# Sixteen drains on GpSimd's queue taken out of a fused attention and mixture-of-experts kernel

## The chip, the cores and the metric

The kernel runs on one core of a Trainium2 chip. Its time is device microseconds of one execution; a measurement is the median of several. A core has four computing engines, each with its own queue of instructions: TensorE (PE, matmul), VectorE (DVE), ScalarE (ACT) and GpSimd (POOL); SyncE (SP) issues transfers. The engines wait for one another by semaphores, and the program sets each of these waits by hand.

## The reference

```
scores = z @ z^T / S                       # per batch, B = 8, S = 3072, 64 features
attn   = max(scores, 0) ** 2
x      = u * (attn @ v)                    # (B*S, 256)
# mixture of experts, E = 8, capacity = 768, F = 1024
expert = argmax(x @ w_gate);  gate = softmax probability of that expert
# the first 768 tokens of an expert, in order, get a place; the others give zero rows
h = max(disp[e] @ w1[e], 0);  y = h @ w2[e]
out[token] = gate * y[its place]
```

## The kernel before

The work has two stages.

The first stage goes over groups of 384 tokens (three tiles of 128). For each group TensorE makes scores and the weighted sums of v, ScalarE and VectorE turn scores into squared weights in two half-precision parts, and the group is routed: VectorE works out each token's place in the buffer `disp`, and GpSimd writes the three tiles of rows there with three indirect DMAs (scatters, line 358). The stage stops early, by a flag that every engine reads, as soon as all experts are full; in these runs that is after 18 groups, so after 54 scatters. In each turn GpSimd waits for the group's places, issues the three scatters, reads the flag, waits until the scatters have landed (`scattered`, line 375) and goes on.

The second stage is a loop of four turns over pairs of experts; each turn has four blocks k = 0 to 3, a block being 384 rows of `disp`. SP loads a block's rows by a transposing DMA and its tail (gate factor and token number) by a plain one (lines 321 and 323), four blocks ahead at first and then each as soon as the scatters of the block that used the buffer have landed (`y_scattered`, line 336). TensorE multiplies by w1 and w2. ScalarE evacuates a block's three result tiles (line 536) and counts `y_ready`; GpSimd waits for each and scatters the tile to `out` (line 393), three scatters for a block and 48 in all. In blocks k = 1 and 3 of the first three turns GpSimd also does an all-reduce over partitions ahead of the scatters (line 388).

Of the kernel before, what the change touches and what calls it, by code (L numbers as in the profile page):

```python
# [40 lines left out]
def relu2_attention_moe(nc, u, v, z, w_gate, w1, w2, out, disp, capacity):  # L41
    B, S, D = u.shape
    DQK = z.shape[2]
    E, _, F = w1.shape
    NG = B * GPB
    DC = D // P
# [10 lines left out]
    with ExitStack() as ctx:  # L57
# [139 lines left out]
        def wait_apart(eng, semaphore, value):  # L197

            eng.wait_ge(semaphore, value)
            if not isinstance(value, int):  # L200
                eng.sem_inc(s["passed"], 1)

        def only_if(eng, cond, step):
            if isinstance(cond, bool):
                if cond:
                    step()
            else:
                with eng.If(cond):
                    step()

        def attention_loop(eng, body):

            end = eng.alloc_register(f"end_{eng.engine.name}")
            eng.reg_mov(end, NG + 1)
            body(0, end)
            with eng.Fori(1, end) as n:
                body(nc.s_assert_within(n, 1, NG), end)

        def load_end(eng, n, end):  # L220

            if isinstance(n, int):
                return
            wait_apart(eng, s["flag_ready"], n)
            eng.reg_load(end, ends[0:1, bass.ds((n - 1) & (NG - 1), 1)])
# [114 lines left out]
        @block.gpsimd  # L340
        def _(pool):
            pool.wait_ge(s["nrm0"], 1)
            pool.partition_all_reduce(amx[:, 0:1], mx[:, 0:1], P, RMAX).then_inc(s["amx0"], 1)
            pool.wait_ge(s["vsum0"], 1)
            pool.partition_all_reduce(amx[:, 1:2], mx[:, 1:2], P, RMAX).then_inc(s["amx0"], 1)
            pool.wait_ge(s["gmx_ready"], 1)
            pool.partition_all_reduce(gamx[:, :], gmx[:, :], P, RMAX).then_inc(s["gamx_ready"], 1)

            def body(n, end):
                g = n & 7  # L350
                if isinstance(n, int):

                    pool.wait_ge(s["disp_filled"], 16 * 8)
                    pool.sem_inc(s["row_free"], 1)
                    return
                wait_apart(pool, s["slot_ready"], n * 2)
                for t in range(TILES):
                    pool.indirect_dma_start(  # L358
                        out=disp[:, :], out_offset=bass.IndirectOffsetOnAxis(ap=slot[:, t:t + 1], axis=0),
                        in_=xrow[:, t, :], in_offset=None, bounds_check=E * capacity - 1, oob_is_err=False,  # L360
                    ).then_inc(s["scattered"], 16)

                def reduce_maxes():
                    wait_apart(pool, s["maxes_ready"], (n & 120) + 8)
                    pool.partition_all_reduce(amx[:, :], mx[:, :], P, RMAX).then_inc(s["allmax_ready"], 8)
                load_end(pool, n, end)
                def all_w(e):
                    pool.wait_ge(s["wmax_ready"], e + 1)
                    pool.partition_all_reduce(wamx[:, :], wmx[:, :], P, RMAX).then_inc(s["wallmax_ready"], 1)

                def rest():
                    only_if(pool, g == 3, reduce_maxes)
                    only_if(pool, n == 8, lambda: all_w(0))
                    only_if(pool, n == 9, lambda: all_w(1))
                wait_apart(pool, s["scattered"], n * 48)
                pool.sem_inc(s["row_free"], 1)
                only_if(pool, pool.snap(end) > 0, rest)
            attention_loop(pool, body)
            pool.drain()
            pool.wait_ge(s["out_zeroed"], 16 * 8)  # L380

            with pool.Fori(0, E // 2) as i:
                for k in range(4):
                    j = i * 4 + k
                    if k % 2:
                        def all_w():
                            wait_apart(pool, s["wmax_ready"], i * 2 + k // 2 + 3)
                            pool.partition_all_reduce(wamx[:, :], wmx[:, :], P, RMAX).then_inc(s["wallmax_ready"], 1)
                        only_if(pool, i < E // 2 - 1, all_w)
                    for at, t in enumerate(BANK_ORDER):  # L390

                        wait_apart(pool, s["y_ready"], j * TILES + TILES + at + 1)
                        pool.indirect_dma_start(  # L393
                            out=out, out_offset=bass.IndirectOffsetOnAxis(
                                ap=tail[:, k, t, 1:2].bitcast(U32), axis=0),
                            in_=ybuf[:, k % 2, t, :], in_offset=None, bounds_check=B * S - 1, oob_is_err=False,
                        ).then_inc(s[f"y_scattered{k}"], 16)
                    only_if(pool, True if k < 3 else i < E // 2 - 1, lambda: pool.drain())
            for k in range(4):
                pool.wait_ge(s[f"y_scattered{k}"], 16 * TILES * E * HALVES // 4)  # L400

# [891 lines left out]
```

## Time and profile before

| | us |
|---|---|
| median of 3 runs | 894.89 |
| lowest and highest | 893.61 and 895.44 |
| the profiled execution | 893.61 |
| its span, first to last instruction | 891.8 |

| engine | busy us | share of the span |
|---|---|---|
| TensorE, matmul | 871.2 | 98% |
| VectorE | 644.3 | 72% |
| ScalarE | 567.0 | 64% |
| GpSimd | 121.5 | 14% |

### The profile page before, as it was taken

Reading aid. Unit: us, or ns where it says so; the run is one execution under the profiler, and the core shown is the slowest. Engines: PE = TensorE matmul, PEld = TensorE weight load, DVE = VectorE, ACT = ScalarE, POOL = GpSimd, SP = SyncE. Lnnn points to the kernel's source line nnn. Section 1 sums busy time; section 2 is a strip of 40 time slices with the busy share of each in tenths; the row PEclk is TensorE's granted clock in tenths of the full one; section 3 lists DMA queues with packets and bytes.
Section 4 is the critical chain, followed back from the end, with each engine's and each line's share of the span. In section 5 each row is a group of like instructions: output and inputs, shape, how many; then the busy total and the mean of one; then the engine's idle time right before and its main releaser. Section 6 shows DMA issues by size and latency. Waiting matters only on the chain.

```text
span 891.8 us, 23154 instructions
## 1 busy us (share of the span) xinstructions
PE 871.2 (98%) x7573; PEld 701.0 (79%) x7574; DVE 644.3 (72%) x1393; ACT 567.0 (64%) x869; POOL 121.5 (14%) x120
## 2 busy tenths in 40 slices
PE   5999999999999999999999999999899999999997
PEld 4787888888888888888888888888677777777775
DVE  7976877988988988889888797677255565655531
ACT  6868786767777679886776777677144344434422
POOL 0001102101101110110110110110112112121212
PEclk9999999999999999999999999999999999999999
DMA  9973528623632740010111112400715245325101
GB/s 269 209 232 129 177 70 295 194 93 101 194 127 67 238 147 7 34 35 18 35 40 31 35 51 61 143 24 18 167 40 149 54 129 165 98 79 152 51 19 36
DMA packets 123207, 93.93 MB, mean 105 GB/s; under 512 B 59453, under 2 KB 118026, under 8 KB 123184
## 3 DMA queue, kind: packets, MB, share of 16 engines
q1 hardware_dynamic: 118288, 80.99, 32.7%
q0 software_dynamic: 4896, 12.64, 4.0%
q8 instruction: 14, 0.23, 0.1%
q14 instruction: 9, 0.07, 0.0%
HBM read 40.03 MB, written 44.93 MB: 95 GB/s over the span
## 4 chain that ended last, share of the span: by engine, by line
PE 95%; DMA 1%; DVE 1%; issue 1%; ACT 0%; POOL 0%; POOLq 0%; SPq 0%; DVEq 0%
PE O L621 16%; PE O L625 16%; PE O L623 16%; PE Sc L740 14%; PE Sc L589 8%; PE Sc L590 8%; PE O L761 5%; PE O L763 5%; PE O L765 5%; PE M L662 1%; DMA vS<-disp 1%; PE M L670 1%; DMA rawz<-in_z 1%; DVE zsq L863 0%; DVE zsq L868 0%
## 5 line engine op out<-in xcount | busy, mean ns | idle before, releaser
L623 PE MATMUL O<-vS,attn_hi 128*128 128x256 f16 x1326 | 361.8, 273 | 0.0
L621 PE MATMUL O<-vS,attn_hi 128*128 128x256 f16 x1326 | 361.7, 273 | 0.0
L625 PE MATMUL O<-vS,attn_lo 128*128 128x256 f16 x1326 | 361.7, 273 | 0.0
L431 ACT ACTIVATE Sc<-Sc 128x768 f32<-128x768 f32 x223 | 177.3, 795 | 78.6 <-PE Sc L590 65.1
L902 DVE TENSOR_TENSOR attn_lo<-attn,attn_hi 128x768 f16<-128x768 f32 x223 | 213.8, 959 | 7.7
L435 ACT ACTIVATE attn<-Sc 128x768 f32<-128x768 f32 x223 | 180.9, 811 | 7.1
L621 PEld LDWEIGHTS O<-vS,attn_hi 128*128 128x128 f16 x1326 | 129.8, 98 | 26.7 <-issue 0.2
L623 PEld LDWEIGHTS O<-vS,attn_hi 128*128 128x128 f16 x1326 | 129.8, 98 | 26.6 <-issue 0.2
L589 PE MATMUL Sc<-zPQ 128*128 (+1 forms) x448 | 146.9, 328 | 3.6 <-ACT attn L435 2.7
L590 PE MATMUL Sc<-zPQ 128*128 (+1 forms) x448 | 147.0, 329 | 0.0
L896 DVE CAST attn_hi<-attn 128x768 f16<-128x768 f32 x223 | 124.4, 558 | 28.0 <-ACT attn L435 22.8
L1206 DVE SCALAR_TENSOR_TENSOR rawv<-Sc,rawv 128x768 f16<-128x768 f32 x64 | 61.2, 956 | 114.3 <-ACT rawv L524 96.6
L625 PEld LDWEIGHTS O<-vS,attn_lo 128*128 128x128 f16 x1326 | 129.8, 98 | 15.3
L358 POOL DMA_INDIRECT disp<-xrow,slot x54 | 69.1, 1280 | 481.2 <-DVE slot L1076 448.0
L524 ACT ACTIVATE rawv<-Sc 128x768 f16<-128x768 f32 x64 | 51.9, 811 | 109.5 <-PE Sc L740 106.2
L740 PE MATMUL Sc<-vS,w1h 128*128 128x384 f16 x512 | 104.1, 326 | 2.2 <-DMA vS<-disp 2.1
L761 PE MATMUL O<-w2s,rawv 128*128 128x256 f16 x384 | 104.7, 273 | 0.0
L763 PE MATMUL O<-w2s,rawv 128*128 128x256 f16 x384 | 104.7, 273 | 0.0
L765 PE MATMUL O<-w2s,rawv 128*128 128x256 f16 x384 | 104.7, 273 | 0.0
L740 PEld LDWEIGHTS Sc<-vS,w1h 128*128 128x128 f16 x512 | 49.9, 98 | 30.7 <-DMA vS<-disp 2.3
L393 POOL DMA_INDIRECT out<-attn,vS x48 | 47.0, 979 | 130.9 <-ACT attn L536 120.2
L589 PEld LDWEIGHTS Sc<-zPQ 128*128 128x128 f16 (+1 forms) x448 | 44.0, 98 | 22.5 <-issue 4.7
(136 smaller groups left out, 823.3 us busy)
## 6 DMA issues: line engine op xcount, KB each, us to landing
out<-empty SPq DMA_DIRECT2D x8, 3072.0 KB
wraw<-in_moe_w SPq DMA_DIRECT2D x16, 1024.0 KB
rawv<-in_v SPq DMA_DIRECT2D x16, 768.0 KB, 8.3
ubuf<-in_u SPq DMA_DIRECT2D x19, 384.0 KB, 3.2
disp<-empty SPq DMA_DIRECT2D x8, 774.0 KB, 17.0
rawz<-in_z SPq DMA_DIRECT2D x3, 768.0 KB
disp<-xrow,slot POOLq DMA_INDIRECT x54
rawz<-in_z SPq DMA_DIRECT2D x2, 384.0 KB, 4.3
```

The lines of the kernel that those rows point to most:

```text
L431: act.activation(pair, pair, ACT.Relu).then_inc(s["relu_done"], 1)
L435: act.activation(attn[:, c % BUFS, :, :], Sp[:, 2 * (c % 2):2 * (c % 2) + 2, 0:GROUP], ACT.Square, scale=ROOT_C).then_inc(s["square_done"], 1)
L589: nc.tensor.matmul(to, keys, zall[:, bass.ds(qb, GROUP)], start=True, stop=False)
L590: ins = nc.tensor.matmul(to, keys, zall[:, bass.ds(qb + SLICE * P, GROUP)], start=False, stop=True)
L621: nc.tensor.matmul(o_part(t), hi, v[:, 0:D], start=c == 0 and j == 0 and t % 2 == 0, stop=False, skip_group_check=True)
L623: nc.tensor.matmul(o_part(t), hi, v[:, D:2 * D], start=False, stop=False, skip_group_check=True)
L625: ins = nc.tensor.matmul(o_part(t), lo, v[:, 0:D], start=False, stop=c == PAIRS - 1 and j == 1, skip_group_check=True)
L740: ins = nc.tensor.matmul(Sp[:, 2 * (p % 2) + fi, 0:GROUP], w[par][:, m, f * P:(f + 1) * P], xt[:, k, x + m, :], start=(at == 0), stop=(at ...
L761: nc.tensor.matmul(o_part(t), hi, w2s[:, par, f, 0:D], start=f == 0 and t % 2 == 0, stop=False, skip_group_check=True)
L763: nc.tensor.matmul(o_part(t), hi, w2s[:, par, f, D:2 * D], start=False, stop=False, skip_group_check=True)
L765: ins = nc.tensor.matmul(o_part(t), lo, w2s[:, par, f, 0:D], start=False, stop=f == FC - 1, skip_group_check=True)
L902: dve.tensor_tensor(attn_lo[:, b, :, :], attn[:, b, :, :], attn_hi[:, b, :, :], ALU.subtract).then_inc(s["lo_done"], 1)
```

## The change

Both drains in the program's text go: the one between the stages, and the one behind each block's scatters together with its condition. All waits on semaphores stay.

```diff
--- before.py
+++ after.py
@@ -376,7 +376,6 @@
                 pool.sem_inc(s["row_free"], 1)
                 only_if(pool, pool.snap(end) > 0, rest)
             attention_loop(pool, body)
-            pool.drain()
             pool.wait_ge(s["out_zeroed"], 16 * 8)
 
             with pool.Fori(0, E // 2) as i:
@@ -395,7 +394,6 @@
                                 ap=tail[:, k, t, 1:2].bitcast(U32), axis=0),
                             in_=ybuf[:, k % 2, t, :], in_offset=None, bounds_check=B * S - 1, oob_is_err=False,
                         ).then_inc(s[f"y_scattered{k}"], 16)
-                    only_if(pool, True if k < 3 else i < E // 2 - 1, lambda: pool.drain())
             for k in range(4):
                 pool.wait_ge(s[f"y_scattered{k}"], 16 * TILES * E * HALVES // 4)
```

## Rows read from the trace of the kernel before

**Rows 1.** The page: TensorE's busy time, and the chain by engine

```profile
PE 871.2 (98%) x7573; PEld 701.0 (79%) x7574; DVE 644.3 (72%) x1393; ACT 567.0 (64%) x869; POOL 121.5 (14%) x120
...
PE 95%; DMA 1%; DVE 1%; issue 1%; ACT 0%; POOL 0%; POOLq 0%; SPq 0%; DVEq 0%
```

**Rows 2.** Stretches: from:to, length, busy by engine, clock, DMA share, GB/s

```profile
0.00:627.00 627.00, 615.27 (x5572) 508.79 (x5574) 515.03 (x1220) 465.06 (x729) 71.68 (x66) 0.99 0.37 109
...
636.00:886.00 250.00, 249.81 (x1914) 186.85 (x1912) 129.02 (x172) 101.17 (x139) 47.19 (x52) 1.00 0.35 96
886.00:891.80 5.80, 0.00 (x0) 0.00 (x0) 0.00 (x0) 0.81 (x2) 1.95 (x2) 0.75 0.19 68
```

**Rows 3.** The chain in order of time, its end: start us, us, what

```profile
885.82 0.12 PE O L765
...
887.33 0.52 POOL out L393
...
888.60 0.98 POOL out L393
```

**Rows 4.** By line, GpSimd's last waits and drains: count, ns min/median/max, first/last start

```profile
L400 POOLq EVENT_SEMAPHORE  x1: 43/43/43, 891.0 to 891.0; - x1
...
L57 POOLq DRAIN  x1: 293/293/293, 891.3 to 891.3; - x1
...
L1279 POOLq DRAIN  x1: 174/174/174, 0.3 to 0.3; - x1
```

**Rows 5.** GpSimd between the stages (timeline, then by line), and all L398 drains

```profile
626.66 0.97 POOL L358 DMA_INDIRECT disp<-xrow,slot  x1 [0.30 <-issue]
...
L201 POOLq EVENT_SEMAPHORE  x1: 17/17/17, 628.8 to 628.8; - x1
...
L379 POOLq DRAIN  x1: 4476/4476/4476, 629.4 to 629.4; - x1
...
L398 POOLq DRAIN  x15: 3368/3392/4001, 656.7 to 875.9; - x15
```

**Rows 6.** By line: three single L398 drains, and SP's waits for scatters' landing

```profile
L398 POOLq DRAIN  x1: 3377/3377/3377, 656.7 to 656.7; - x1
L201 SPq EVENT_SEMAPHORE  x1: 17/17/17, 659.9 to 659.9; - x1
...
L398 POOLq DRAIN  x1: 4001/4001/4001, 674.7 to 674.7; - x1
...
L398 POOLq DRAIN  x1: 3617/3617/3617, 688.0 to 688.0; - x1
L201 SPq EVENT_SEMAPHORE  x1: 17/17/17, 691.5 to 691.5; - x1
```

**Rows 7.** Timeline of GpSimd, second stage: start, us, what [idle before <-releaser]; one wait

```profile
653.96 0.97 POOL L393 DMA_INDIRECT out<-attn,vS  x1 [26.33 <-ACT attn L536]
...
672.15 0.36 POOL L388 PARTITION_ALL_REDUCE wamx<-wmx  x1 [13.66 <-DVE wmx L1168]
...
685.27 0.97 POOL L393 DMA_INDIRECT out<-attn,vS  x1 [8.22 <-ACT attn L536]
...
L201 POOLq EVENT_SEMAPHORE  x1: 17/17/17, 883.9 to 883.9; - x1
...
884.79 0.97 POOL L393 DMA_INDIRECT out<-attn,vS  x1 [7.06 <-ACT attn L536]
```

**Rows 8.** By line, GpSimd's scatters of either stage, ns min/median/max

```profile
L358 POOL DMA_INDIRECT disp<-xrow,slot x54: 974/1182/1528, 69.6 to 626.7; - x54
...
L393 POOL DMA_INDIRECT out<-attn,vS x48: 967/972/1027, 654.0 to 888.6; - x48
```

**Rows 9.** Seam: TensorE's wait (by waits), landing of loads issued at 629.3 and 660.1

```profile
PE Sc L740 <- DMA vS<-disp: 2.1, 1, 2.1
...
DMA to landing us min/median/max: 5.4/5.4/5.4
...
DMA to landing us min/median/max: 3.6/3.6/3.6
```

## The prediction

> **What bounds the kernel now.** I read the shares of the engines and of the chain first [rows 1]: TensorE is busy 98% of the span and 95% of the chain is TensorE, so the body of the kernel goes at the pace of the matmuls. GpSimd is busy 14%, and the edit touches GpSimd alone. The table of stretches [rows 2] says the same by stage: from 636 to 886 us TensorE is busy 249.8 of 250 us; the 5.8 us after 886 have no matmul in them. So I read two places instruction by instruction: this end, and the seam between the two stages, where TensorE waits 2.1 us once [rows 9].
>
> The end [rows 3]: the last matmul stands there until 885.94, ScalarE evacuates, GpSimd issues its second scatter at 887.33 and its third at 888.60, which ends at 889.58. The chain stops there, 2.2 us ahead of the span's end. That is the row on which this forecast hangs.
>
> **The change, part by part.** It removes L379 (one drain, 4.476 us) and L398 (15 drains, 3.37 to 4.00 us each) [rows 5], with the condition around the one in k = 3, and adds nothing.
>
> *What the drains cost where they stand: nothing.* L379 runs from 629.4 to 633.9 (629.4 + 4.476), and the next thing GpSimd does is the scatter at 653.96, which waited 26.3 us for ScalarE [rows 7]: 19 us of cover. For L398 I took the three kinds of place. Behind k = 0 the drain ends at 660.1 (656.7 + 3.38), and the all-reduce that is next waits for VectorE until 672.15; behind k = 1 it ends at 678.7, and the next scatter, at 685.27, waited for ScalarE; behind the last k = 2 it ends at 879.3 (875.9 + 3.37), and GpSimd's wait passes at 883.9 [rows 5 to 7]. The smallest cover is 4.6 us, so no drain delays a scatter. Gain from removing the waits: 0.0. Nobody waits for the drains either: SP waits for the landing of the scatters (y_scattered), not for GpSimd's queue. GpSimd issues nothing else behind them than the all-reduce and scatters of the next block, which wait for VectorE and ScalarE in any case. The branch that goes in k = 3 lies, in the last turn, beside the last scatters and the 1.5 us in which the third lands (889.58 to 891.0, [rows 3, 4]): 0.0 as well.
>
> *What the drains do: here I see work, not only waiting.* Compare L379 with L57. Before both, GpSimd's last scatter had ended some 1.7 us earlier (626.66 + 0.97 = 627.6 against 629.4; 889.6 against 891.3), and both stand behind a wait for its landing (628.8 and 891.0). Neither has anything left to wait for. Yet one takes 4.476 us and the other 0.293 [rows 4, 5]. What differs is how many scatters were issued since the last drain: 54 against 3 (L358 has 54, L393 has 48, [rows 8], and the last group of three has no drain behind it). If a drain has a bookkeeping cost for every scatter not yet drained, a fixed part a and b each: a + 3b = 293 and a + 54b = 4476, so b = 4183 / 51 = 82 ns and a = 47 ns.
>
> Two rows can't test a line of two unknowns, so I looked for a third. The L398 drains wait for the landing of their third scatter: 656.7 + 3.377 = 660.08, and SP, which waits for that same landing, passes at 659.9; 688.0 + 3.617 = 691.6 against 691.5, where the landing was late and the drain late with it [rows 6]. If earlier scatters are done while it waits, one is left at the landing: 47 + 82 = 129 ns. Seen: 0.1 to 0.2 us. It fits.
>
> *What is late next.* With the 16 drains gone, L57's is the first since the start, with 54 + 48 = 102 scatters behind it: 47 + 102 x 82 = 8.41 us in place of 0.293, so +8.12 us, all on the path, because nothing else runs then.
>
> Bounds of this unknown. Above: at L57's own rate, 293 / 3 = 98 ns a scatter, 9.96 us, so +9.67. Below: if the 4.476 us is a price of the first large drain whatever its number, +4.18; if L57 stays what it is, 0; and below nothing, the 1.8 us of the faster rival. I take the line of both rows.
>
> *The scatters themselves.* In the first stage, with no drains in it, they take a median of 1182 ns, in the second, with drains, 972 [rows 8]. If the drains are why, two of the last three would each be 0.21 us longer on the path: at most +0.4. In the first stage VectorE is far busier (515 of 627 us against 129 of 250, [rows 2]), and the last scatter of that stage, at 626.66 and with 53 undrained ones before it, took 0.97 [rows 5]; I take 0 and keep 0.4 for the range.
>
> *Sum.* The profiled execution took 893.61 (span 891.8 and 1.8 around it). 893.61 + 0 + 8.12 = 901.7. It was the fastest of the three runs; their mean is 894.65, so the forecast for a median is 894.65 + 8.12 = 902.8 us, 0.9% slower.
>
> The Trainium skill speaks against it. Its page "PSUM — Partial Sum Buffer", section "Engine vs sequencer instructions", says that a drain waits until the engine is wholly idle. By that rule L379, issued 1.7 us after the engine's last work, would have been over at once, and the time would stay where it is; the row of 4.476 us disagrees. The page "DMA: Bandwidth & Descriptors", section "SWDGE vs HWDGE vs iDMA", says that GpSimd's cores append the descriptors of their DMAs to rings in SBUF; no row shows these rings, but slots that must be taken back would be a cost per scatter, as the rows have it.
>
> **The rivals.**
> *R1, the drain only waits (not slower).* L379's 4.476 us is then something of its place: SP issues its first eight loads in a row from 629.3 on, and the first lands 5.4 us after its issue, where a lone one takes 3.6 [rows 9], so something was crowded there. L57 stands alone in either kernel and stays 0.29: 893.61 + 0, 894.6 for a median. For it: one long drain is all there is. Against it: 0.29 against 4.48 with the engine idle before both, and the third check. It decides if L57 in the new trace is under 0.5 us. The skill's sentence above is this rival.
> *R2, the cost is there but not 102-fold.* A first drain after long use is slow once (4.476), or what the drain works off has a limit and the scatters themselves pay beyond it. Then L57 is about 4.5 us: 894.65 + 4.18 = 898.8. For it: nothing excludes it. Against it: the drain at the very start took 174 ns [rows 4], with no scatter before it; and the 54th undrained scatter was as quick as any.
> *R3, faster.* The L379 drain and the first load of expert rows run together (629.4 to 633.9; issued at 629.3). If the drain is what crowds that load, its landing comes 5.4 - 3.6 = 1.8 us earlier, TensorE's wait of 2.1 us there shrinks by as much [rows 9], and with L57 unchanged the end comes at 894.65 - 1.8 = 892.8. Against it: seven other loads stand behind that one in SP's queue, which crowd it without any drain. If the drain did both, R3 takes 1.8 off the main case: 901.0, inside the range.
>
> **How the numbers follow.** Main case 0.72, R2 0.10, R1 0.14, R3 0.04. The prediction is the main case's, 902.8. Its own range is 901.0 (with R3's gain) to 904.8 (+9.67 and +0.4), and the three runs spread by 0.8 above their mean and 1.0 below. The range must reach into R2 to hold 8 in 10: 898.0 to 905.5. What of the time a measurement can't tell from no change is about 0.2%, 1.8 us. Slower by more than that: main and R2, 0.82; within: R1, 0.14; faster: R3, which lies at its edge, 0.04.
>
> **What would show it.** In GpSimd's queue at the end, L57's DRAIN: 8.4 us confirms the line, 4.5 R2, 0.3 R1. The wait for the last landing should pass 1.5 us after the last scatter's end, as now; TensorE's wait at the seam should stay at 2.1 us, and the stretch from 636 to 886 as full. The forecast is wrong at its root if the last drain is short; wrong in size if it is long but far from 8.4; and wrong in "free where they stand" if a scatter starts sooner behind its wait than now: at the end its wait passes at 883.9 and the scatter starts at 884.79 [rows 7].

## The result and the profile after

| | us |
|---|---|
| before, median of 5 runs | 893.61 (892.01 to 895.44) |
| after, median of 5 runs | 901.79 (900.02 to 903.05) |
| ratio | 1.0088, 95% interval 1.0073 to 1.0103 |
| the profiled execution after | 902.05, span 900.3 |

The kernel is 0.9% slower: 7.9 us by the ratio. The prediction was slower by 8.1 us, 902.8 in a range of 898.0 to 905.5.

The page and the stretches of the kernel after, with the columns of [rows 1] and [rows 2]:

```profile
PE 871.3 (97%) x7573; PEld 700.8 (78%) x7574; DVE 644.1 (72%) x1393; ACT 566.6 (63%) x869; POOL 121.3 (13%) x120
```

```profile
0.00:627.00 627.00, 614.90 (x5563) 508.21 (x5565) 514.88 (x1220) 464.78 (x729) 71.27 (x65) 0.99 0.38 109
...
637.00:887.00 250.00, 249.19 (x1910) 186.42 (x1908) 128.97 (x172) 101.69 (x140) 47.09 (x52) 1.00 0.35 96
887.00:900.30 13.30, 0.00 (x0) 0.00 (x0) 0.00 (x0) 0.18 (x1) 1.94 (x2) 0.62 0.06 21
```

Every engine has the busy time it had. What is longer is the stretch behind the last scatter, in which nothing that counts as busy happens. GpSimd's last instructions, by line (count, ns min/median/max, first and last start), and its timeline:

```profile
L398 POOLq EVENT_SEMAPHORE  x2: 17/30/43, 888.3 to 891.4; - x2
...
L57 POOLq DRAIN  x1: 8396/8396/8396, 891.6 to 891.6; - x1
```

```profile
885.16 0.97 POOL L392 DMA_INDIRECT out<-attn,vS  x1 [7.07 <-ACT attn L534]
887.69 0.97 POOL L392 DMA_INDIRECT out<-attn,vS  x1 [1.56 <-ACT attn L534]
888.97 0.97 POOL L392 DMA_INDIRECT out<-attn,vS  x1 [0.30 <-issue]
```

The last scatter ends at 889.94 and has landed by 891.4 (L398 is the last wait here, two lines less than L400), as far apart as before, 889.58 and 891.0 [rows 3, 4]. Then the drain at the end of the block takes 8.396 us, where it took 0.293 [rows 4]. That is 8.10 of the 8.5 us by which the span grew. The other 0.4 has nothing to do with the drains: the first scatter of all is already 0.6 us late, 70.14 against 69.57 before, and from there to the end the lag stays between 0.4 and 0.6. Between 24 and 38 us the granted clock was 0.91 here and 0.95 in the profile before, which would account for it.

The seam is as it was, in TensorE's wait and in the landing of the first load, with no drain beside it [rows 9]:

```profile
PE Sc L738 <- DMA vS<-disp: 2.1, 1, 2.1
...
DMA to landing us min/median/max: 5.3/5.3/5.3
```

So are the scatters of either stage, drained or not [rows 8]:

```profile
L392 POOL DMA_INDIRECT out<-attn,vS x48: 963/972/1026, 654.3 to 889.0; - x48
...
L358 POOL DMA_INDIRECT disp<-xrow,slot x54: 972/1183/1530, 70.1 to 627.1; - x54
```

### The profile page after: what moved, and what is told of

It is laid out like the page before. It is cut to its first block, busy times and chain, and to the rows that moved or that the text cites. A ratio compares the mean times of both kernels' runs of the same rounds, so it can differ in the third digit from the quotient of the medians.

```text
span 900.3 us, 23134 instructions
## 1 busy us (share of the span) xinstructions
PE 871.3 (97%) x7573; PEld 700.8 (78%) x7574; DVE 644.1 (72%) x1393; ACT 566.6 (63%) x869; POOL 121.3 (13%) x120
## 4 chain that ended last, share of the span: by engine, by line
PE 94%; DMA 1%; DVE 1%; issue 1%; ACT 0%; POOL 0%; POOLq 0%; SPq 0%; DVEq 0%
PE O L619 16%; PE O L621 16%; PE O L623 16%; PE Sc L738 14%; PE Sc L587 8%; PE Sc L588 8%; PE O L759 5%; PE O L763 5%; PE O L761 5%; PE M L660 1%; DMA vS<-disp 1%; PE M L668 1%; DMA rawz<-in_z 1%; DVE zsq L861 0%; DVE zsq L866 0%
```

## The experiments

The theory going in: a drain on GpSimd costs a fixed 47 ns (40 in the later expectations, after the first experiment) and 82 ns for each DMA that GpSimd has issued since its last drain. Against it: a first long drain whatever the number (R2), a price of the place (R1), a cost by rows. All edits are to the kernel after. Where an interval stands, the time is a ratio to the kernel before on the same chip, from ten or more executions; the other kernels were run once, and their verdict is the drain's duration alone.

**Drain between the stages put back, twice.**

```diff
             attention_loop(pool, body)
+            pool.drain()
+            pool.drain()
             pool.wait_ge(s["out_zeroed"], 16 * 8)
```

> The changed kernel with the drain between the stages put back, and a second drain directly behind it; none behind the blocks. Backlog theory (a drain costs 47 ns plus 82 ns for each scatter issued since the last drain): first drain 4.48 us for 54 scatters, the second only the fixed part, 0.05 us, the last one (L57) 47 + 48 x 82 = 3.98 us; time about 3.7 us above the kernel before. First-drain theory (R2, a long first drain whatever the number): first 4.48, L57 back at 0.3, time as before. If 4.48 belongs to its place beside SP's loads: the second drain is long too, since the loads are still running.

Measured: ratio 1.0034 (1.0025 to 1.0044), so +3.0 us (2.2 to 3.9), where 3.7 was expected. GpSimd's drains by line:

```profile
L379 POOLq DRAIN  x1: 4476/4476/4476, 629.9 to 629.9; - x1
...
L380 POOLq DRAIN  x1: 40/40/40, 634.4 to 634.4; - x1
...
L57 POOLq DRAIN  x1: 3983/3983/3983, 891.7 to 891.7; - x1
```

The second drain stands in the same place, with the same loads of SP running, and takes 40 ns: the place is not what costs, and the fixed part is 40 ns. The last one has 48 scatters behind it and takes 3.98: being first is not it either. A drain pays for what came before it and leaves the next one free of it.

**A drain inside the first stage.**

```diff
                 pool.sem_inc(s["row_free"], 1)
+                only_if(pool, n == 8, lambda: pool.drain())
...
             attention_loop(pool, body)
+            pool.drain()
```

> The changed kernel with the drain between the stages put back and one more inside the first stage, after group 8's scatters have landed (24 scatters so far); none behind the blocks. Backlog theory: 47 + 24 x 82 = 2.02 us in the loop, 47 + 30 x 82 = 2.51 us between the stages (at the very place where 54 scatters gave 4.48), L57 3.98 us. Place theory: the drain between the stages stays 4.5 us. First-drain theory: the one in the loop is 4.5 us and both others are short.

```profile
L377 POOLq DRAIN  x1: 2031/2031/2031, 308.7 to 308.7; - x1
...
L380 POOLq DRAIN  x1: 2508/2508/2508, 630.6 to 630.6; - x1
...
L57 POOLq DRAIN  x1: 3973/3973/3973, 893.5 to 893.5; - x1
```

2.03, 2.51 and 3.97 us against 2.02, 2.51 and 3.98 expected. At the very place of the 4.476 us, 30 scatters in place of 54 give 2.508. (The time of this one execution, 899.56, holds some 2 us that are no drain's: the last matmul ended at 888.2 instead of 885.9. Of these 2.3 us, 1.0 is there ahead of the drain in the loop, where a scatter starts at 299.01 against 297.97 before. The rest comes behind the seam: the last scatter of the first stage starts at 627.68 against 626.66, still 1.0 late, and the first of the second stage at 656.24 against 653.96. Between 636 and 640 us the granted clock was 0.60, against 1.00 before and 1.00 in the kernel with two drains at that place.)

**One drain, late.**

```diff
                         ).then_inc(s[f"y_scattered{k}"], 16)
+                    if k == 2:
+                        only_if(pool, i > E // 2 - 2, lambda: pool.drain())
```

> The changed kernel with a single drain, behind block k = 2 of the last turn, where the cover between its issue (875.9) and GpSimd's next release (883.9) is 8.0 us; 99 scatters stand before it. Backlog theory, if the drain works the backlog off while its last scatter still flies: 47 + 99 x 82 = 8.2 us from issue, it ends about when the next wait passes, L57 is 0.29 us again, and the time is that of the kernel before within 0.3 us. If it begins only once the last scatter has landed (879.2), it ends at 887.3, all three last scatters are late and the time is 2.5 to 3.5 us above before. If a single late drain can't pay for all, L57 is long: up to 8 us above.

Measured: ratio 1.0009 (0.9995 to 1.0022). The drains by line, GpSimd's timeline, and the head of the chain from 883 us:

```profile
L398 POOLq DRAIN  x1: 9871/9871/9871, 873.5 to 873.5; - x1
...
L57 POOLq DRAIN  x1: 298/298/298, 889.7 to 889.7; - x1
```

```profile
874.21 0.97 POOL L392 DMA_INDIRECT out<-attn,vS  x1 [0.30 <-issue]
884.48 0.97 POOL L392 DMA_INDIRECT out<-attn,vS  x1 [9.29 <-ACT attn L536]
885.75 0.97 POOL L392 DMA_INDIRECT out<-attn,vS  x1 [0.30 <-issue]
```

```profile
875.19 8.19 issue
883.38 0.04 POOLq L208
```

The drain is longer than the 8.2 us expected from its issue, and shorter than if it began at the landing; the chain says why. The drain was issued at 873.48, before the third scatter of its block ran, and its own work begins when that scatter's instruction ends, at 875.19: from there to the drain's end at 883.35 it is 8.16 us, and 40 + 99 x 82 ns is 8.16. (The chain's 8.19 reaches to the next instruction.) It doesn't wait for the landing first: that comes about 1.4 us behind the instruction's end, and the drain would have ended as much later. With it the cover is gone: ScalarE had evacuated the first tile at 880.90 + 0.47, and the scatter that should start 0.9 us behind that starts at 884.48, 2.2 us late. The row names ScalarE as releaser; the chain names GpSimd's own queue, and the chain is right. The next scatter runs 0.30 behind it, and the end comes about 1 us late: from the last matmul's end to the third scatter's it is 4.6 us here (883.4 to 888.0) and 3.65 before (885.9 to 889.6). This is the price of one block too late. Only the profile shows it; the interval of the time reaches from 0.4 us faster to 2.0 us slower.

**One drain, one block earlier.**

```diff
-                    if k == 2:
+                    if k == 1:
```

> The changed kernel with a single drain, one block earlier than in the run with one late drain: behind k = 1 of the last turn, 96 scatters before it. If the drain's own work starts when the last scatter's instruction has ended (about 862.1) it lasts 40 + 96 x 82 ns = 7.9 us and ends at 870.0, 2 us before GpSimd's next release at 872.0: no scatter is late. L57 has 6 scatters, 0.53 us against 0.29: 0.24 us above the kernel before, which can't be told from it in time. If the cost does not move with the drain, L57 stays near 8 us and the time 8 us above.

Measured: ratio 1.0004 (0.9994 to 1.0014).

```profile
L398 POOLq DRAIN  x1: 9622/9622/9622, 860.5 to 860.5; - x1
...
L57 POOLq DRAIN  x1: 543/543/543, 891.4 to 891.4; - x1
```

```profile
861.24 0.97 POOL L392 DMA_INDIRECT out<-attn,vS  x1 [0.30 <-issue]
873.01 0.97 POOL L392 DMA_INDIRECT out<-attn,vS  x1 [10.80 <-ACT attn L536]
```

From the scatter's end (862.21) to the drain's (870.13) it is 7.92 us for 96 scatters, as expected, and it is over 2 us before the next release. The last drain has six scatters, 0.543. One drain in the whole program does what sixteen did, as far as the times can tell. They can't tell this place from the one a block later either: the two intervals overlap.

**By scatter or by row.**

```diff
-                                ap=tail[:, k, t, 1:2].bitcast(U32), axis=0),
-                            in_=ybuf[:, k % 2, t, :], in_offset=None, ...
+                                ap=tail[0:64, k, t, 1:2].bitcast(U32), axis=0),
+                            in_=ybuf[0:64, k % 2, t, :], in_offset=None, ...
```

> The changed kernel with the 48 scatters of the second stage writing only 64 of their 128 rows (the upper half of each tile is left out of the output). Tells whether the cost is by scatter or by row. By scatter: L57 stays at 8.4 us. By row or descriptor: 54 x 82 + 48 x 41 + 47 ns = 6.4 us.

```profile
L57 POOLq DRAIN  x1: 8396/8396/8396, 891.1 to 891.1; - x1
...
L392 POOL DMA_INDIRECT out<-attn,vS x48: 902/906/922, 653.9 to 888.5; - x48
```

This kernel leaves half the rows of each tile out of the output. Its last drain takes the same 8396 ns to the nanosecond. The scatter's own instruction is a little shorter with 64 rows (906 against 972), the drain isn't: it goes by the scatter.

**Do plain DMAs count?**

```diff
+                    pool.dma_start(scr[:, :, :], w_gate.rearrange(...)).then_inc(s["scr_loaded"], 16)
+                    wait_apart(pool, s["scr_loaded"], j * 16 + 16)
```

> The changed kernel with one plain (not indirect) load of 8 KB added to GpSimd's queue behind each block's scatters, each waited for: 16 of them, 102 scatters as before. If every DMA that GpSimd issues counts alike: L57 = 40 ns + 118 x 82 = 9.7 us. If only indirect ones count: 8.4 us. If by rows or descriptors, anything else, but the halved rows have shown no such share.

It gave 5.292 us, far below both values: a miss of all that I had on the table. And two scatters stood out, one late and the next one long. The last drain by line, and GpSimd's timeline there:

```profile
L57 POOLq DRAIN  x1: 5292/5292/5292, 892.1 to 892.1; - x1
...
841.74 1.03 POOL L393 DMA_INDIRECT out<-attn,vS  x1 [7.84 <-ACT attn L537]
845.38 0.98 POOL L393 DMA_INDIRECT out<-attn,vS  x1 [2.61 <-issue]
846.66 1.69 POOL L393 DMA_INDIRECT out<-attn,vS  x1 [0.31 <-issue]
```

These are the 103rd to 105th DMA since the start. Two more kernels were made for it: the same with the drain between the stages put back, and one with three plain loads for each block (each with a buffer of its own).

```diff
             attention_loop(pool, body)
+            pool.drain()
```

> The run with 16 added plain loads gave L57 = 5.29 us, neither of the two values expected, and its 105th DMA since the last drain took 1.69 us instead of 0.97. Here the same kernel with the drain between the stages put back, so that only 48 scatters and 16 plain loads stand before L57. If plain loads count as scatters do: 40 + 64 x 82 ns = 5.29 us. If they count for nothing: 3.98. No DMA should be long, since the backlog never passes 64.

```diff
-                    pool.dma_start(scr[:, :, :], ...).then_inc(s["scr_loaded"], 16)
-                    wait_apart(pool, s["scr_loaded"], j * 16 + 16)
+                    for q in range(3):
+                        pool.dma_start(scr[:, q, :, :], ...).then_inc(s["scr_loaded"], 16)
+                    wait_apart(pool, s["scr_loaded"], j * 48 + 48)
```

> The changed kernel with three plain loads behind each block, so 54 + 48 + 48 = 150 DMAs of GpSimd with no drain. If a backlog of 104 is a limit and the next DMA then takes back 54 of them within its own 0.7 us (118 - 54 = 64 gave 5.29): a long DMA again at the 105th, none later (150 - 54 = 96), and L57 = 40 + 96 x 82 ns = 7.9 us. If the long one was chance and unrelated: L57 = 150 x 82 ns = 12.3 us.

With the drain between the stages, 48 scatters and 16 plain loads gave 5.285, which is 64 DMAs (40 + 64 x 82 = 5.29), and the same stretch was undisturbed:

```profile
L57 POOLq DRAIN  x1: 5285/5285/5285, 892.3 to 892.3; - x1
...
841.93 1.03 POOL L394 DMA_INDIRECT out<-attn,vS  x1 [7.83 <-ACT attn L538]
844.19 0.98 POOL L394 DMA_INDIRECT out<-attn,vS  x1 [1.23 <-ACT attn L538]
845.48 0.97 POOL L394 DMA_INDIRECT out<-attn,vS  x1 [0.31 <-issue]
```

So plain DMAs count as scatters do, and by the same price the 5.292 was a backlog of 64 out of 118: 54 were no longer there. I read this as GpSimd having taken them back on the way; no row shows it doing so. With 150 DMAs my 7.9 was wrong: 2.761 us, 33 DMAs' worth, so 117 were gone. Wrong too was the long DMA at the 105th: the 103rd to 105th (from 777.66 on) are as quick as any, though nothing gave the 104th more time: the idle ahead of it is 1.20 us, and 1.23 in the undisturbed stretch above. The late scatter was the 134th:

```profile
L57 POOLq DRAIN  x1: 2761/2761/2761, 892.3 to 892.3; - x1
...
779.92 1.02 POOL L393 DMA_INDIRECT out<-attn,vS  x1 [1.20 <-ACT attn L539]
...
855.62 1.05 POOL L393 DMA_INDIRECT out<-attn,vS  x1 [8.54 <-ACT attn L539]
859.80 1.02 POOL L393 DMA_INDIRECT out<-attn,vS  x1 [3.13 <-issue]
```

Last, two plain loads for each block (`range(2)` and `j * 32 + 32` in the edit above), and the first of these kernels, unchanged, once more:

> The changed kernel with two plain loads behind each block: 54 + 48 + 32 = 134 DMAs of GpSimd, no drain. With 102 the last drain was 8.40 us, with 118 it was 5.29 (64 DMAs' worth) and a stretch around the 104th DMA was about 2 us late; with 150 it was 2.76 (33 worth) and the second scatter of one block (the 134th DMA) about 1.6 us late. If the DMAs take back the backlog themselves once it is somewhere over 103: a late scatter again between the 103rd and the 134th, and L57 well under the 11.0 us of 134. If those two runs were odd and the line goes on: 11.0 us.

> The run with 16 added plain loads once more. If its 5.29 us and its late 104th and 105th DMA are a property of the program: the same again within 0.05 us. If chance of that run: 9.7 us.

134 DMAs gave 6.599 us: 80 DMAs' worth, 134 - 54. No scatter was late there, so one half of that expectation failed. The repeat gave 5.292 again, with the same scatter late by the same 2.61 us of idle: it is the program's, not chance's.

All drains with a known backlog, where GpSimd's engine had nothing left to execute when the drain's work began, against 40 ns + 82 ns each:

| DMAs since the last drain | the drain, us | 40 + 82 n |
|---|---|---|
| 0 | 0.040 | 0.04 |
| 3 | 0.293, 0.298 | 0.29 |
| 6 | 0.543 | 0.53 |
| 24 | 2.031 | 2.01 |
| 30 | 2.508 | 2.50 |
| 48 | 3.983, 3.973 | 3.98 |
| 54 | 4.476 | 4.47 |
| 64 (48 scatters, 16 plain) | 5.285 | 5.29 |
| 102 | 8.396 | 8.40 |

The drain at the very start of the program, 174 ns with no DMA before it [rows 4], is not in the table: GpSimd's last memset still ran until 0.45 us, and it started at 0.3.

## Why the prediction was right

*Nothing gained where the drains stood*: right. 653.96 became 654.32 and 884.79 became 885.16, both by the 0.4 us of lag that the execution had from its first scatter on, and the wait at the end stands as far ahead of its scatter as before (884.3 to 885.16).

*A drain does work by the number of scatters*: right, and now shown, where the prediction had two rows and a rough third. The second drain of 40 ns at the crowded seam and the 2.508 us for 30 scatters at the same place rule out the place (R1). The 3.98 us of a drain that was not the first rules out a once-only price (R2's first half).

*+8.12 us on the path*: measured +8.10 in the drain itself and +7.9 in the ratio. The fixed part is 40 ns, not 47. The forecast of the time itself, 902.8 against 901.79, stood on a mean before of 894.65, and the median before was 893.61 in the measurement: the change came out as forecast, and the starting point was 1.0 us high. (The upper end of the range's own sum, 894.65 + 9.67 + 0.4, is 904.7 and not 904.8.)

*The check by the block drains*: its conclusion holds, its picture needed one correction. I had them work off earlier scatters while they wait. The single late drain shows that the work starts at the end of the last scatter's instruction and not at the drain's issue, and the block drains show that the landing, if it is later, is waited for besides: they end 0.1 to 0.2 us after it. How much of the three scatters' 0.25 us is done before the landing is not shown, so that the sum of 129 ns came near this was weak support.

*Scatters longer without drains (at most +0.4)*: no. 972 ns in both kernels.

*R2's second half, a limit beyond which the scatters themselves pay*: it was not reached at 102, so it played no part in the result, but beyond 102 something of this kind exists. With 118 and 134 DMAs 54 were gone from the last drain, with 150 it was 117. A scatter paid for it in two programs (1.4 us late at the 104th, 1.6 us at the 134th) and none in the third. What sets these amounts, and at which DMA it begins, stays open; the number of DMAs alone doesn't set it, since the 104th was late in one program and not in another, where it had no more idle time ahead of it.

*R3, faster*: no. The first load at the seam lands after 5.3 us instead of 5.4, with no drain beside it.

No kernel here beats the one before. Its last drain is down to 0.293 us, of which 0.25 is for the last three scatters; this is all that a better placing of drains could still win, and it was not tried, being far under what a measurement can tell.

## What to carry to other kernels

A drain can be payment and not a wait: before taking one out, look at what the next one on that engine will cost, the one at the end of the block above all, since nothing hides it. On GpSimd each DMA since the last drain cost 82 ns there (up to 102 of them), so a kernel that ends soon after its last GpSimd DMA wants one drain in an idle stretch before the end, long enough for the whole backlog (8 us for 100 DMAs), counted from the end of the DMA instruction ahead of it. And an instruction that appears in no busy time and in no group of the page can be the longest thing on the path: look up what fills the time between the end of the chain and the end of the span.

## What the runs showed of the hardware that was not expected

- GpSimd's drain costs 40 ns + 82 ns for each DMA issued since the last one, up to the 102 of the table, the same for scatters of 128 or 64 rows (8396 ns both) and for plain loads of 8 KB (5.285 us for 64 of mixed kind), and the engine being idle makes it no shorter. The Trainium skill's sentence that a drain waits until the engine is wholly idle ("PSUM — Partial Sum Buffer", section "Engine vs sequencer instructions") is not the whole of it on this engine: the trace has 8.396 us with the engine idle for 1.7 us before.
- With more than 102 undrained DMAs the last drain was shorter than their number asks: by 54 of 118 (the same in a repeat), by 54 of 134, by 117 of 150. That GpSimd takes the missing part back itself, between its DMAs, is my reading of this and of the two late scatters.
- None of this cost is seen on other engines. Their drains at the end of the block, in the kernel after (by line; PEld is TensorE's sequencer):

```profile
L57 SPq DRAIN  x1: 13/13/13, 837.5 to 837.5; - x1
L57 DVEq DRAIN  x1: 24/24/24, 882.8 to 882.8; - x1
L57 PEldq DRAIN  x1: 1922/1922/1922, 884.4 to 884.4; - x1
L57 ACTq DRAIN  x1: 866/866/866, 886.4 to 886.4; - x1
```

SP, the only other engine that issues DMAs here, has issued all its loads by then, with no drain behind any of them, and pays 13 ns. TensorE's and ScalarE's are long while their last work still runs: they end at 886.3 and 887.3, and the last matmul and the last evacuation end at 886.3 and 887.2.
